# Attention scores as stacked high and low f32r products, with queries and keys split on chip, in a kernel of top-k attention and two feed-forward layers

## What is computed

```python
def _attn_ref(q, k, v):                       # (2, 8, 576, 64) each
    scores = np.matmul(q, k.transpose(0, 1, 3, 2)) / np.sqrt(D)
    kth = np.partition(scores, -32, axis=-1)[..., -32:-31]
    scores = np.where(scores >= kth, scores, -1e9)
    attn = softmax(scores)                    # 32 of 576 keys stay in each row
    return np.matmul(attn, v)

x = attn_out as (1152 tokens, 512)            # tokens of both batches
P = sinkhorn(x @ w_gate)                      # 8 rounds over (1152, 8)
x = sum_e P[:, e:e+1] * (relu(x @ w1[e]) @ w2[e])       # 8 experts, 512 -> 1024 -> 512
h = x @ w_in; out = (h * tanh(softplus(h))) @ w_out     # 512 -> 2048 -> 512
```

## Time and profile before

| | before |
|---|---|
| time, median of 3 runs | 1380.41 us (1378.27 to 1384.98) |
| time of the profiled execution | 1380.37 us |
| its span (first to last instruction) | 1378.6 us |
| mean granted PE clock | 0.985 |
| busy: PE, PEld | 1349.0 us (98%), 1165.1 us (85%) |
| busy: DVE, ACT, POOL | 753.9 (55%), 619.8 (45%), 447.1 us (32%) |

### The profile page before, as it was taken

How to read it: one execution, slowest core, us unless ns; L and a number is a source line. 1 busy time by engine, 2 the same in 40 slices (tenths; PEclk the granted TensorE clock), 3 DMA queues, 4 the chain that set the end, 5 groups by cost and what they waited for, 6 DMA issues and landing times.

```text
span 1378.6 us, 20129 instructions
## 1 busy us (share of the span) xinstructions
PE 1349.0 (98%) x7219; PEld 1165.1 (85%) x7219; DVE 753.9 (55%) x1375; ACT 619.8 (45%) x1154; POOL 447.1 (32%) x254
## 2 busy tenths in 40 slices
PE   7989999999999999999999999999999999999998
PEld 5877878788888889989998888999998888889776
DVE  4978967777788783044331313131322224788776
ACT  3444455656666565342222222222222223888776
POOL 1223444445454546773222233222222231000000
PEclk8998999999999999999999999999999999999999
DMA  8020012222222133341313222122212111122231
GB/s 134 17 73 9 18 53 85 92 75 95 85 84 99 62 99 100 107 142 50 115 51 95 66 78 83 62 88 70 85 61 84 61 62 62 61 77 72 82 115 47
DMA packets 139699, 105.27 MB, mean 76 GB/s; under 512 B 34288, under 2 KB 116208, under 8 KB 139632
## 3 DMA queue, kind: packets, MB, share of 16 engines
q1 hardware_dynamic: 139632, 104.37, 24.8%
HBM read 96.49 MB, written 7.86 MB: 76 GB/s over the span
## 4 chain that ended last, share of the span: by engine, by line
PE 88%; ACT 6%; DVE 4%; issue 1%; DMA 0%; SPq 0%; POOL 0%; DVEq 0%
PE ps L501 30%; PE ps L516 30%; PE ps L446 7%; PE ps L425 6%; PE ps L529 4%; PE ps L733 3%; PE ps L711 3%; PE ps L436 3%; ACT m_d L936 1%; ACT m_r L939 1%; ACT m_a L934 1%; ACT m_r L941 1%; DVE m_r L1163 1%; DVE m_a L1160 1%; DVE m_a L1166 1%; ACT h_hi L948 1%
## 5 line engine op out<-in xcount | busy, mean ns | idle before, releaser
L1270 POOL TENSOR_TENSOR w_lo<-w_raw,w_hi 128x1024 fp32r<-128x1024 f32 x130 | 314.2, 2417 | 416.8 <-ACT w_hi L763 416.8
L1092 DVE SCALAR_TENSOR_TENSOR h_lo<-ps,h_hi 128x384 fp32r<-128x384 f32 x128 | 71.1, 557 | 362.2 <-ACT h_hi L909 362.2
L501 PE MATMUL ps<-x_hi,w_hi 128*128 128x384 f32 x768 | 265.2, 345 | 0.0
L501 PE MATMUL ps<-x_hi,w_lo 128*128 128x384 f32 x768 | 260.3, 339 | 0.0
L501 PE MATMUL ps<-x_lo,w_hi 128*128 128x384 f32 x768 | 259.3, 338 | 0.0
L909 ACT ACTIVATE h_hi<-ps 128x384 fp32r<-128x384 f32 x128 | 62.9, 492 | 401.5 <-PE ps L501 401.5
L763 ACT ACTIVATE w_hi<-w_raw 128x1024 fp32r<-128x1024 f32 x160 | 168.3, 1053 | 3.8 <-DMA w_raw<-in_moe_w 3.6
L501 PEld LDWEIGHTS ps<-x_hi,w_hi 128*128 128x128 f32 x768 | 144.7, 188 | 21.0 <-issue 10.5
L516 PE MATMUL ps<-w_hi,h_hi 128*128 128x512 f32 x384 | 152.5, 397 | 0.0
L1005 DVE MAX8 top<-work 128x8 f32<-128x576 f32 x216 | 152.4, 747 | 0.0
L516 PE MATMUL ps<-w_hi,h_lo 128*128 128x512 f32 x384 | 151.4, 394 | 0.0
(11 more groups left out here) (113 smaller groups left out, 2258.0 us busy)
## 6 DMA issues: line engine op xcount, KB each, us to landing
w_raw<-in_moe_w SPq DMA_DIRECT2D x256, 256.0 KB, 2.9
w_raw<-in_moe_w_in SPq DMA_DIRECT2D x32, 256.0 KB, 2.7
w_raw<-in_moe_w_out SPq DMA_DIRECT2D x32, 256.0 KB, 3.0
spill<-y_out SPq DMA_DIRECT2D x7, 768.0 KB, 3.8
y_in<-spill SPq DMA_DIRECT2D x7, 768.0 KB, 4.4
qraw<-in_q SPq DMA_DIRECT2D x18, 128.0 KB, 3.1
vones<-in_v SPq DMA_DIRECT2D x8, 256.0 KB, 5.1
out<-acc SPq DMA_DIRECT2D x8, 256.0 KB, 2.9
```

The source lines that it names most:

```text
L501: last = nc.tensor.matmul(ps[:, bank, 0:BT], wt[:, s, 0, c * P:(c + 1) * P], xt[:, c, blk * BT:(blk + 1) * BT], start=(n == 0), stop=(n == ...
L1092: v_.scalar_tensor_tensor(out=h_lo[:, s, :], in0=ps[:, HB_BANK + j, 0:BT], scalar=0.0, in1=h_hi[:, s, :], op0=ALU.max, op1=ALU.subtract).t ...
L1270: g_.tensor_tensor(w_lo[:, s, :, :].rearrange("p a n -> p (a n)"), w_raw[:, s, :, :].rearrange("p a n -> p (a n)"), w_hi[:, s, :, :].rearr ...
```

## The change

- `scores`: each of the two halves of a head is now two accumulating f32r matmuls on 128 rows. `q_s[:, 0]` holds, for one head, the queries' high part on 64 rows and the low part on the other 64, `q_s[:, 1]` the two the other way round; `k_s` holds high above low. The two products together are high x high + low x low + low x high + high x low. In tile 4 the first batch's 64 rows are computed after the second's, whose matmul writes all 128 rows first.
- Transposes: a tile's queries take 16 transposes in four groups `r` (two orders of the parts, two halves of the heads) in place of 4: groups 0 and 1 at h = 5 and 6 of the tile before, groups 2 and 3 at h = 0 and 1 of the tile itself, behind `up_a`. A key block takes 8 in place of 4. In tile 0 the heads 4 to 7 of the keys and the query groups 2 and 3 are transposed between the first four heads' scores (`first_keys`).
- Splits: ACT writes the high parts (two copies for the queries, one per key block), DVE the low parts of tile 0's queries and batch 0's keys, POOL all others, between its masks. ACT copies four query groups per tile in place of one, and two groups per key block, DVE two of those of batch 0. (The high and low parts of the keys, `key_parts`, lie in the weights' buffers `w_hi` and `w_lo`.)
- `keep_clock`, called after the scores of 28 heads (tiles 0 to 2 and the first four of tile 3), is gone, with nothing in its place.
- Transfers: keys land in the weights' buffers and in `y_out`, each block in a place of its own, so all ten are loaded without a wait; the first weights wait until the keys' low parts are made; the queries for tile T + 1 wait until tile T's four groups are transposed.

```diff
-        kraw = sb("kraw", [P, 2, DM], where=early)
-        kT = sb("kT", [P, B, NPAIR, S], where=early)
+        k_s = sb("k_s", [P, B, H, S], F32R, where=early)
         vones = sb("vones", [P, B, KC, H, DV], where=early)
-        qraw = sb("qraw", [P, H, D], where=early)
-        qT = sb("qT", [P, NPAIR, P], where=early)
+        q_parts = sb("q_parts", [P, H, 3, D], F32R, where=early)
+        q_s = sb("q_s", [P, 2, H, P], F32R, where=early)
...
+            def next_queries(T, low, high):
+                sp.wait_ge(q_tr, 4 * T)
+                load_queries(low, high)
...
+            def keys_transposed(b, c, g):
                 n = P if c < TB else REST
-                j = b * KC + c
-                pe.wait_ge(k_in[key_slot(j)], 16 * (1 if j < KC else (j - KC) // 2 + 2))
-                if j == 1:
-                    pe.wait_ge(q_copied, 1)
-                elif j >= 2:
-                    pe.wait_ge(k_copied, j - 1 if j < KC else j)
-                for p in range(NPAIR):
-                    last = nc.tensor.transpose(ps[:, key_bank(j), p * P:p * P + n],
-                                               raw_keys(j, n)[:, p * P:(p + 1) * P], ident[0:n, 0:n])
+                parts = key_parts(b, c).bitcast(F32)
+                for i in range(HH):
+                    last = nc.tensor.transpose(ps[:, KEY_BANKS[b, g][c], i * P:i * P + n],
+                                               parts[:, g * HH + i, :, :].rearrange("p a d -> p (a d)"),
+                                               ident[0:n, 0:n])
                 last.then_inc(k_tr, 1)
 
-            def queries_transposed(T, first=False):
-                pe.wait_ge(q_in, 32 * T + 32)
-                if not first:
-                    pe.wait_ge(pt_copied, head(T - 1, 4) + FREE)
-                for p in range(NPAIR):
-                    last = nc.tensor.transpose(ps[:, PT_BANK, p * P:(p + 1) * P],
-                                               qraw[:, 2 * p:2 * p + 2, :].rearrange("p h d -> p (h d)"),
-                                               ident[:, :])
+            def queries_transposed(T, r):
+
+                for i in range(HH):
+                    last = nc.tensor.transpose(ps[:, query_bank(T, r), i * P:(i + 1) * P],
+                                               q_parts[:, r // 2 * HH + i, r % 2:r % 2 + 2, :].bitcast(F32).rearrange(
...
             def scores(T, h, parts):
+
                 pe.wait_ge(s_copied, head(T, h) + FREE)
-                o = D * (h % 2)
                 for j in range(2):
-                    for b, r, n in parts:
-                        last = nc.tensor.matmul(ps[r:r + n, S_BANK + j, 0:HALF], qT[o:o + D, h // 2, r:r + n],
-                                                kT[o:o + D, b, h // 2, j * HALF:(j + 1) * HALF],
-                                                start=True, stop=True)
+                    for b, r, n in reversed(parts):
+                        for part in range(2):
+                            last = nc.tensor.matmul(ps[0:r + n, S_BANK + j, 0:HALF], q_s[:, part, h, 0:r + n],
+                                                    k_s[:, b, h, j * HALF:(j + 1) * HALF],
+                                                    start=(part == 0), stop=(part == 1))
                 last.then_inc(s_ready, 1)
...
-                    else:
-                        keep_clock()
-                    if following and h == H - 1:
-                        queries_transposed(T + 1)
-                    if isinstance(T, int) and T == 0 and h == 4:
+                    if h in (0, 1) and not first:
+                        pe.wait_ge(pt_copied, head(T - 1, h + 4) + 1 + FREE)
+                        queries_transposed(T, h + 2)
+                    if h in (5, 6) and following:
+                        pe.wait_ge(pt_copied, head(T, h - 4) + 1 + FREE)
+                        pe.wait_ge(q_low, T + 1)
+                        queries_transposed(T + 1, h - 5)
...
+                        pe.wait_ge(k_high, KC + h)
+                        pe.wait_ge(k_low1, h)
+                        if h == 1:
+                            pe.wait_ge(q_copied, 4)
+                        else:
+                            pe.wait_ge(k_copied, KEYS_0 + 2 * h - 2)
+                        keys_transposed(1, h - 1, 0)
+                        keys_transposed(1, h - 1, 1)
...
-            def keep_clock():
-
-                for _ in range(FILLERS):
-                    nc.tensor.matmul(ps[:, YA_BANK, 0:P], ones[:, :], ident[:, :], start=True, stop=True)
...
+            pe.wait_ge(q_low0, 1)
+            queries_transposed(0, 0)
+            queries_transposed(0, 1)
             for c in range(KC):
-                keys_transposed(0, c)
-            pe.wait_ge(k_copied, KC)
+                pe.wait_ge(k_low0, c + 1)
+                if c == 2 or c == 3:
+                    pe.wait_ge(q_copied, c - 1)
+                elif c == 4:
+                    pe.wait_ge(k_copied, 1)
+                keys_transposed(0, c, 0)
+            pe.wait_ge(q_copied, 2)
+            pe.wait_ge(k_copied, KEYS_FIRST)
+            pe.wait_ge(k_copied_d, len(BY_DVE))
...
+            def keys_high(b, c):
+                act.wait_ge(k_in[b * KC + c], 16)
+                if b * KC + c >= 2 * RING:
+                    act.wait_ge(k_tr, b * KC + c - 2 * RING + 1)
+                copy(key_parts(b, c)[:, :, 0, :],
+                     raw_keys(b, c).rearrange("p (h d) -> p h d", h=H)).then_inc(k_high, 1)
+
+            def keys_copied(b, c, g):
+                act.wait_ge(k_tr, KC * g + c + 1 if b == 0 else 2 * KC + 2 * c + g + 1)
+                copy(key_place(b, c, g), key_columns(c, KEY_BANKS[b, g][c])).then_inc(k_copied, 1)
+
+            def queries_high(T):
+                act.wait_ge(q_in, 32 * T + 32)
+                copy(q_parts[:, :, 0, :], raw_queries())
+                copy(q_parts[:, :, 2, :], raw_queries()).then_inc(q_high, 1)
+
+            def queries_copied(T, r):
+                act.wait_ge(q_tr, 4 * T + r + 1)
+                copy(q_s[:, r % 2, r // 2 * HH:(r // 2 + 1) * HH, :].rearrange("p a n -> p (a n)"),
+                     ps[:, query_bank(T, r), :]).then_inc(q_copied, 1)
...
-                        queries_copied(T + 1)
+                    if h in (0, 1) and not first:
+                        queries_copied(T, h + 2)
+                    if h in (5, 6) and following:
+                        queries_copied(T + 1, h - 5)
                     if late_on:
                         output_copied(late, (h - 4) % H, two_before if h < 4 else before)
+                    if h == (4 if first else 3) and following:
+                        queries_high(T + 1)
...
+            queries_high(0)
+            keys_high(0, 0)
+            keys_high(0, 1)
+            queries_copied(0, 0)
+            keys_high(0, 2)
+            queries_copied(0, 1)
+            keys_copied(0, 0, 0)
+            keys_high(0, 3)
+            keys_copied(0, 2, 0)
+            keys_high(0, 4)
+            keys_copied(0, 3, 0)
...
+            def first_queries_low():
+                dve.wait_ge(q_high, 1)
+                v_.tensor_tensor(raw_queries(), raw_queries(), q_parts[:, :, 0, :], ALU.subtract).then_inc(q_low0, 1)
+
+            def keys_low(c):
+                dve.wait_ge(k_high, c + 1)
+                parts = key_parts(0, c)
+                v_.tensor_tensor(parts[:, :, 1, :], raw_keys(0, c).rearrange("p (h d) -> p h d", h=H),
+                                 parts[:, :, 0, :], ALU.subtract).then_inc(k_low0, 1)
+
+            def keys_copied(c):
+                dve.wait_ge(k_tr, c + 1)
+                v_.tensor_copy(key_place(0, c, 0), key_columns(c, KEY_BANKS[0, 0][c])).then_inc(k_copied_d, 1)
+
+            first_queries_low()
+            for c in range(3):
+                keys_low(c)
+            keys_copied(1)
+            keys_low(3)
+            keys_low(4)
+            keys_copied(4)
...
+            def queries_low(T):
+                pool.wait_ge(q_high, T + 1)
+                g_.tensor_tensor(raw_queries(), raw_queries(), q_parts[:, :, 0, :], ALU.subtract).then_inc(q_low, 1)
...
-                for h in range(1, H, 2):
-                    mask(T, h)
+                mask(T, 1)
+                queries_low(T + 1)
+                mask(T, 3)
+                if T == 0:
+                    keys_low(0)
+                    keys_low(1)
+                mask(T, 5)
+                if T == 0:
+                    keys_low(2)
+                    keys_low(3)
+                mask(T, 7)
+                if T == 0:
+                    keys_low(4)
```

More of the change, by code:

```diff
@@ L307, in load_queries @@
             def load_queries(low, high):
-                sp.dma_start(qraw[0:REST], q_v[low[0], bass.ds(low[1], REST)]).then_inc(q_in, 16)
-                sp.dma_start(qraw[REST:P], q_v[high[0], bass.ds(high[1], REST)]).then_inc(q_in, 16)
+                sp.dma_start(raw_queries(slice(0, REST)), q_v[low[0], bass.ds(low[1], REST)]).then_inc(q_in, 16)
```

(42 more changed lines are left out.)

119 lines of the change are left out of this document (72 added, 47 removed).

## The result

| | before | after |
|---|---|---|
| time, median of 4 runs each | 1379.88 us | 1333.64 us (1333.43 to 1334.47) |
| span of the profiled execution | 1378.6 us | 1331.7 us |
| busy PE, DVE, ACT, POOL | 1349.0, 753.9, 619.8, 447.1 us | 1283.2, 766.8, 645.2, 464.3 us |
| mean granted PE clock | 0.985 | 0.961 |

The ratio is 0.966, with an interval of 0.9634 to 0.9686: faster, by 46 us. The profiled execution took 1333.57 us.

The account below looks back on a forecast made before the run. DVE's selection, held up by PE's fillers, was to bound tiles 1 and 2, and PE the chunk stage. -29.7 - 2.3 + 6.6 - 16 - 1 - 1.2 = -43.6 us gave 1337 us, range 1329 to 1359.

Parts of the forecast that it names:

- Rival 1: Tile 1: the low clock makes PE the bound, keeping 6 us of its stall, 1343 us; chance 0.13.
- Rival 2: Scores of 43 heads: f32r scores pay the 0.2 us on both sides, 18 us, giving 1355; chance 0.12.
- Rival 4: Chunk stage: the low clock lasts into it, some 5 us more a head, up to 1397 us; chance 0.04.
- Rival 5: Scores: f32r products are not one pass each, 2.3 us a head, +73 us, 1410; chance 0.03.
- Rival 3: Early tiles: DVE's wait for the row sums stays, as latency over four engines, 1345 us; chance 0.08.
- -29.7: Chunk stage, 35 heads: f32r scores and the twelve matmuls behind them take 0.85 us less a head, -29.7 us.
- -2.3: Mixed tile, eight heads: f32r scores save 0.29 us a head, -2.3 us.
- +6.6: From tile 3's head 5 on: 15 more groups of query transposes at 0.44 us each, +6.6 us.
- 0.22 us is a cost of following f32 products: Chunk stage: the twelve matmuls take 2.31 us behind f32 scores, 2.09 us behind transposes without f32 scores between.
- both come through PE, which stands behind its own fillers: Early tiles: DVE's waits for scores and for the last head's output, 19.4 us in all, were put on PE's fillers.
- 4.0 us a head: Early tiles without fillers: PE's time a head even at the low clock, against DVE's 5.2 us.
- -16 - 1 - 1.2: Early part: -16 us of DVE's waits, -1 us at DVE's full start, -1.2 us at head 4 of tile 3.

Follow-up runs that it names:

- experiment 1: Changed kernel with fillers put back behind the scores of the 28 early heads: 8 fillers gave 1334.05 us, 16 gave 1375.14 us.
- experiment 4: Changed kernel with f32 scores over 128 rows in the 36 heads of undivided tiles that have a chunk: 1348.67 us.
- experiment 5: Changed kernel, three runs: chunk f32r scores over 64 rows, 1348.31 us; early f32 scores over 64 rows, 1369.08 us; last value product zero-padded to 128 rows, 1316.43 us.
- the run of 1316.43 us: Changed kernel with the last product of each value product over 128 rows, the upper 64 of them zero: 1316.43 us.
- experiment 2: Kernel before with its fillers taken out and nothing else, 1395.24 us; with 4 fillers instead of 8, 1400.71 us.

## Why the prediction came out, and where its reasons failed

**The time.** 1337.0 was forecast, with 1329 to 1359; it is 1333.6. Of its own signs these came: scores 0.53, the twelve 2.09, a tile 55.4 us, the clock of tiles 1 and 2 at 0.73 and 0.66. DVE's waits were 6.3 us and not near 3, most of them for scores. Rivals 1 and 2 did not happen, nor 4 (PE was at full speed within the first chunk's matmuls) and 5 (four records, 0.53 us). Rival 3 was wrong: the row sums are not waited for unless PE is late, and experiment 1's 16 fillers bring the wait back.

**The chunk stage: right sum, wrong cause.** The terms -29.7, -2.3 and +6.6 give 25.4, and 25.3 was measured. But the step said "0.22 us is a cost of following f32 products". It is a cost of the change between 64 and 128 rows. Type alone gives 15.0 us (experiment 4), rows alone 14.7 (experiment 5); the two add up to the 29.7 that the term had. That the number came out is luck as far as the reason goes: it was right only because the new scores also fill 128 rows, as the neighbours of the earlier trace rows did. And since the step gave the price to the f32 type, it overlooked that the scores themselves held 0.19 us of it, and that the values, untouched by the change, kept paying it on both sides in every head: the 17 us of experiment 5.

**The fillers and the DVE stage: the step that failed.** "DVE should set the pace" came true, "both come through PE, which stands behind its own fillers" did not hold. Put back behind the new scores, the fillers cost nothing; taken from the old ones, their absence cost 16 us. "4.0 us a head" at the low clock was too little as well: it took the values at the 1.60 us of the earlier trace rows, a group in which the clock rose, and they take 2.47 there, so a head is 1.12 + 0.21 + 0.96 + 2.47 = 4.8 us. It stayed under 5.2 and so did no harm. What the runs put in the place of -16 - 1 - 1.2, measured as -21.5:

| early heads' scores | fillers | time |
|---|---|---|
| f32, 64 rows, chunks as before | 8 | 1379 |
| f32, 64 rows, chunks as before | 0 | 1395.2 |
| f32, 64 rows | 0 | 1369.1 |
| f32, 128 rows | 0 | 1335.8 |
| f32r, 128 rows | 0 | 1333.6 |
| f32r, 128 rows | 8 | 1334.1 |
| f32r, 128 rows | 16 | 1375.1 |

The second and third row differ by 26.1 us, the chunk stage's 25.3 and little else, so the rest of the change (loads, keys, start) is worth about 1 us. From 1379: +16 for the fillers, -26 for the chunks, -33 for the rows of the early scores, -2 for their type. Where PE can stay under DVE's 5.2 us a head, these prices vanish, where it can't they are paid, and the late row sums add to them. In the kernel before PE had 5.1 us a head at the full clock, the query and key transposes on top, and the first heads after a turn of a tile at the low level. Its old scores over 128 rows with the 8 fillers were not run, so how the early gain divides there is argued from the rows of this table.

**The start.** Predicted -1 for DVE's full start, against 21.07 us in the earlier trace rows; it came at 18.82, so -2.3, at the good end of the bounds.

## What to carry to other kernels

Look for products that don't fill the 128 rows between ones that do, above all where each side is short: here padding with zeros was faster than not multiplying them, 0.3 to 0.4 us for each such place. When a cost shows only beside one neighbour, list all properties in which that neighbour differs (type, rows, columns, bank) before naming one, and look for the same cost elsewhere in the trace. Whether fillers pay is a question of which engine is a few tenths of a us from being the bound: try them both ways after each change of the work around them.

## What the runs showed of the hardware

- A change between products of 64 and of 128 rows costs PE about 0.2 us at the full clock: 0.19 in front (0.72 against 0.53 us, 1.16 against 0.97) and 0.19 to 0.22 behind (2.28 and 2.31 against 2.09), for f32 and f32r alike, and 0.14 and 0.16 around the values; about 0.3 at the low level. The Trainium skill says in "TensorE: Matmul & The Clock Gate", section "Why this matters for your kernels", that a single product of 32 rows takes the same time as one of 128. No run here has a product by itself; in a stream, experiment 5 shows a difference at the first product on each side of a change, and none among those between.
- The row count doesn't explain every such cost. In the mixed tile of the run of 1316.43 us, `down` still takes 2.27 to 2.30 us behind values of 128 rows whose results fill 64 partitions. Fewer columns of weights alone don't explain it either: in the changed kernel the mixed tile's scores end with f32r products of 64 columns, and the twelve behind them take 2.09 us. The cause is open.
- In the changed kernel PE stayed at the low level (granted 0.50) while it was busy for the whole of 40 to 50 us:

```profile
40.00:50.00 10.00, 10.00 (x43) 9.00 (x42) 10.00 (x22) 6.38 (x16) 5.21 (x5) 0.50 0.00 1
```

It was granted 1.00 from 60 to 70 us, though PE was busy for 7.92 of these 10 us only, 0.50 again from 75 to 80, and 1.00 from 165 us on, after a rise within the first chunk's twelve products.

- The recorded clock can't be trusted alone: in experiment 2 it is 1.00 from 120 to 130 us, where four f32 passes of scores take 2.21 us and not 1.16.
- Four f32r products of 288 columns took 0.53 us, 0.133 each and in one pass, against the 0.131 of the prediction's line through 384 and 512 columns.
